# One tile of the fullest expert taken out of the plan and worked on while the last block is routed

## The reference

```python
h = x @ w_in                    # [2304, 2048]
x2 = (h - np.tanh(h)) @ w_out   # [2304, 512]
xn = x2 / (norm(x2) + 1e-6); en = expert_emb / (norm(expert_emb) + 1e-6)
logits = xn @ en.T / tau
expert_idx = np.argmax(logits, axis=1)
gate_w = softmax(logits)[arange(N), expert_idx]
for e in range(E):
    mask = expert_idx == e
    h = np.maximum(x2[mask] @ w1[e], 0.0)
    out[mask] = gate_w[mask, None] * (h @ w2[e])
```

## Time and profile before

| | us |
|---|---|
| median of 3 runs | 864.16 (864.05 to 864.76) |
| the profiled execution, its own time | 865.77 |
| its span | 863.6 |
| PE busy | 811.5 (94%) |
| DVE / ACT / POOL busy | 473.6 / 367.6 / 199.9 |

### The profile page before, as it was taken

How to read it: one execution, slowest core, us unless ns; L and a number is a source line. 1 busy time by engine, 2 the same in 40 slices (tenths; PEclk the granted TensorE clock), 3 DMA queues, 4 the chain that set the end, 5 groups by cost and what they waited for, 6 DMA issues and landing times. The chain is left out here.

```text
span 863.6 us, 16644 instructions
## 1 busy us (share of the span) xinstructions
PE 811.5 (94%) x4680; PEld 694.1 (80%) x4681; DVE 473.6 (55%) x1399; ACT 367.6 (43%) x910; POOL 199.9 (23%) x276
## 2 busy tenths in 40 slices
PE   7999999999999999999999999399999999999992
PEld 6888888888888888888888998377888888888871
DVE  7666655765577557755774565645533152545312
ACT  5554544433443344334432323325544262655433
POOL 4466521213121221221122000311112111111111
PEclk9999999999999999999999999589999999999996
DMA  9872123221322233222315110146461432566110
GB/s 173 232 233 62 38 50 98 74 60 48 97 68 64 49 87 82 62 49 70 85 26 219 61 50 1 38 120 246 140 218 53 146 134 80 193 231 221 48 43 20
DMA packets 106310, 87.87 MB, mean 102 GB/s; under 512 B 79012, under 2 KB 80169, under 8 KB 106242
## 3 DMA queue, kind: packets, MB, share of 16 engines
q1 hardware_dynamic: 98386, 74.92, 29.4%
q0 software_dynamic: 4624, 11.32, 4.2%
q10 hardware_dynamic: 3232, 0.79, 0.5%
HBM read 152.87 MB, written 11.46 MB: 190 GB/s over the span
## 5 line engine op out<-in xcount | busy, mean ns | idle before, releaser
L1259 PE MATMUL banks<-xh,win_h 128*128 128x384 f32 x384 | 135.5, 353 | 0.6 <-issue 0.6
L710 ACT CAST gh<-gf 128x384 fp32r<-128x384 f32 x96 | 49.2, 513 | 194.1 <-PE banks L1261 172.1
L958 DVE TENSOR_TENSOR gl<-gf,gh 128x384 fp32r<-128x384 f32 x96 | 59.2, 617 | 130.1 <-ACT gh L710 130.1
L1261 PE MATMUL banks<-xh,win_l 128*128 128x384 f32 x384 | 129.3, 337 | 0.0
L1260 PE MATMUL banks<-xl,win_h 128*128 128x384 f32 x384 | 129.1, 336 | 0.0
L1259 PE MATMUL banks<-wout_h,gh 128*128 128x512 f32 x288 | 119.8, 416 | 1.3 <-ACT x L719 1.3
L1260 PE MATMUL banks<-wout_l,gh 128*128 128x512 f32 x288 | 113.5, 394 | 0.0
L1261 PE MATMUL banks<-wout_h,gl 128*128 128x512 f32 x288 | 113.4, 394 | 0.0
L521 POOL TENSOR_TENSOR sm<-sm,rr 128x384 f32<-128x384 f32 x48 | 41.7, 869 | 273.3 <-DVE rr L883 273.2
L703 ACT ACTIVATE gf<-banks 128x384 f32<-128x384 f32 x96 | 46.9, 488 | 105.0 <-PE banks L1261 104.9
L1136 DVE TENSOR_TENSOR hTl<-banks,hTh 128x512 fp32r<-128x512 f32 x50 | 32.3, 686 | 92.1 <-ACT hTh L807 92.0
(11 more groups left out here) (192 smaller groups left out, 1513.5 us busy)
## 6 DMA issues: line engine op xcount, KB each, us to landing
w1raw<-in_moe_w_dram SPq DMA_DIRECT2D x104, 512.0 KB
w2raw<-in_moe_w_dram SPq DMA_DIRECT2D x104, 512.0 KB
x2T<-unit_embeddings SPq DMA_DIRECT2D x20, 256.0 KB, 3.6
junk<-unit_embeddings SPq DMA_DIRECT2D x20, 256.0 KB, 3.4
x_rows<-x SPq DMA_DIRECT2D x6, 768.0 KB, 5.1
wout_raw<-in_moe_w_out_dram SPq DMA_DIRECT2D x4, 1024.0 KB, 6.8
win_raw<-in_moe_w_in_dram SPq DMA_DIRECT2D x3, 1024.0 KB, 9.8
vw<-in_v_dram SPq DMA_DIRECT2D x16, 192.0 KB, 3.3
```

The source lines that it names most:

```text
L710: act.copy(gh[c % 2][:], gf[c % 2][:]).then_inc(g_high, 1)
L958: dve.tensor_tensor(gl[c % 2][:], gf[c % 2][:], gh[c % 2][:], ALU.subtract).then_inc(g_split, 1)
L1259: pe.matmul(to, sh, mh, start=start, stop=False)
L1261: return pe.matmul(to, sl, mh, start=False, stop=stop)
```

## The change

One tile, called the star in the code, leaves the plan. At c = 1 and 2 of the last block PE and DVE count the tokens of blocks 0 to 3 by expert and choose the fullest expert (`choose_star`; there are more than enough tokens for one full tile). SP then loads the first 128 rows of that expert's region of `table` and that expert's w1 and w2, where it loaded expert 0's before; POOL gathers the 128 rows of `x2` at c = 9, PE transposes them at c = 11, ACT and DVE split them at c = 12 and 13. ACT and DVE round and split the star's weights into slot 1, from c = 15 on and between the steps of the last routing; one piece of w2 is subtracted by POOL. PE makes the star's first product in pairs of pieces between the steps of the routing, and its hidden transposes and second product after the counts. Expert 0's w1 is loaded once the star's w1 is split, its w2 once the star's w2 is split. The plan gets one tile less (NTILE = 24), its start in the expert's region moved on by 128 rows (five more small DVE operations before `rows_planned`, one fewer after it). The star's output is scattered after the first two gathers.

```diff
-    NTILE = (T + E * (P - 1)) // P
+    NTILE = (T + E * (P - 1)) // P - 1
...
-        xh = sb("xh", [P, KC, 2, 2, GT], F32R, phase1)
+        xh = sb("xh", [P, 2, KC, 2, GT], F32R, phase1)
...
+        xg, xgh, xgl = [None, None], [None, None], [None, None]
+        for i in (1, 0):
...
-        psJ = banks[:, 0, :]
+        psJ = psXG_star = banks[:, 6, :]
+        psY_star = banks[:, 4, :]
...
-                if s == SLOTS * (NBLK - 1):
+                if s == SLOTS * (NBLK - 1) + 5:
                     sp.wait_ge(attended, NG)
-                    sp.wait_ge(table_cleared, 32)
-                    fetch_w1(None, 0, None)
-                    fetch_w2(None, 0, None)
+                    sp.wait_ge(star_chosen, 1)
+                    e = sp.value_load(star_int[0:1, 0:1], min_val=0, max_val=E - 1)
+                    sp.wait_ge(scattered, 16 * ST * (NBLK - 2))
+                    sp.dma_start(star_rows[:], table.rearrange("(n s) c -> n s c", s=P)[ds(e * MAXT, 1)].rearrange("n s c -> (n s) c")).then_inc(star_rows_loaded, 16)
+                    fetch_w1(None, e, None)
+                    fetch_w2(None, e, None)
                 if n > 0 and at == 7:
                     store(n - 1)
                 if n > 0 and at % 2 == 0 and 0 <= at // 2 - 1 < E:
                     load_en_row(n - 1, at // 2 - 1)
             store(NBLK - 1)
+            sp.wait_ge(star_w1_split, KC)
+            fetch_w1(None, 0, None)
+            sp.wait_ge(star_w2_split, KC - 1)
+            sp.wait_ge(star_w2_split_pool, 1)
+            fetch_w2(None, 0, None)
...
+                    if n == NBLK - 1 and c == 9:
+                        pool.wait_ge(star_ids_ready, 1)
+                        pool.wait_ge(h_ready, FC * (NBLK - 1))
+                        pool.wait_ge(x2_stored, 16 * (NBLK - 1))
...
             pool.wait_ge(squared, ST * NBLK)
             pool.tensor_tensor(norm[:], ss[:], power[:], ALU.pow).then_inc(rooted, 1)
+            pool.wait_ge(star_w2_high, 3)
+            pool.tensor_tensor(w2l4[:, ds(1, 1), 2, :].rearrange("p a f -> p (a f)"), w2raw[:, 2, :],
+                               w2h4[:, ds(1, 1), 2, :].rearrange("p a f -> p (a f)"), ALU.subtract).then_inc(star_w2_split_pool, 1)
             scatter_slots(NBLK - 1)
...
             gather(0, 0, 1)
+            pool.wait_ge(star_y_copied, 1)
+            pool.indirect_dma_start(out=out, out_offset=bass.IndirectOffsetOnAxis(ap=star_ids[:, 0:1], axis=0),
+                                    in_=star_y[:], in_offset=None, bounds_check=T - 1, oob_is_err=False).then_inc(star_y_stored, 16)
...
+            def star_round_w1(pieces):
+                round_w(w1raw, w1_loaded, w1h, ds(1, 1), star_w1_high, 16, pieces)
...
+                    if n == NBLK - 1 and c == FC - 1:
+                        star_round_w1([0])
                     high_g(n, c)
                     pieces(s + 1)
+                    if n == NBLK - 1 and c == 12:
+                        act.wait_ge(star_x_transposed, 1)
+                        act.copy(xgh[1][:], psXG_star.rearrange("p (k t) -> p k t", k=KC)).then_inc(star_x_high, 1)
...
-            round_w(w1raw, w1_loaded, w1h, ds(0, 1), w1_high, 16, [0, 1])
+            star_round_w1([1, 2, 3])
             wait(act, x2_stored, 16 * (NBLK - 1))
             act.wait_ge(dotted, ST * E * (NBLK - 1))
             for st in range(2):
                 act.wait_ge(acc_done, st + 1)
                 act.copy(x2[:, st, :], acc[st]).then_inc(acc_copied, 1)
             act.wait_ge(acc_copied, ST * NBLK)
+            act.wait_ge(star_x_split, 1)
             wait(act, rooted, NBLK - 1)
             for st in range(ST):
                 wait(act, squared, ST * (NBLK - 1) + st)
                 act.activation(psJ, x2[:, st, :], ACT.Square, accum_out=ss[:, st:st + 1]).then_inc(squared, 1)
+            def star_relu(half):
...
+            act.wait_ge(used, NBLK * FC)
+            round_w(w2raw, w2_loaded, w2h4, ds(1, 1), star_w2_high, 16)
+            star_relu(0)
             exp_gate(NBLK - 1)
-            round_w(w1raw, w1_loaded, w1h, ds(0, 1), w1_high, 16, [2, 3])
-            act.wait_ge(used, NBLK * FC)
-            round_w(w2raw, w2_loaded, w2h4, ds(0, 1), w2_high, 16)
+            star_relu(1)
+            for half in range(2):
+                act.wait_ge(star_hid_transposed, half + 1)
+                act.copy(hTh[:, half * KC:(half + 1) * KC, :], psHT[half].rearrange("p (k t) -> p k t", k=KC)).then_inc(star_hT_high, 1)
+            round_w(w1raw, w1_loaded, w1h, ds(0, 1), w1_high, 32)
+            act.wait_ge(star_y_ready, 1)
+            act.wait_ge(x2_stored, 16 * NBLK)
+            act.activation(star_y[:], psY_star, ACT.Copy, scale=star_rows[:, 1:2]).then_inc(star_y_copied, 1)
+            round_w(w2raw, w2_loaded, w2h4, ds(0, 1), w2_high, 32)
...
+            def choose_star():
...
+                then(dve.tensor_copy(count, psN))
...
+                then(dve.tensor_scalar(star[:], em8[:, 0, :], least, None, ALU.is_equal))
+                dve.tensor_scalar(star_int[:], least, float(E), None, ALU.add).then_inc(star_chosen, 1)
...
+            def star_low_w1(pieces):
...
+                    if n == NBLK - 1 and c == FC - 1:
+                        star_low_w1([0])
                     low_g(n, c)
                     pieces(s + 1)
+                    if n == NBLK - 1 and c == 2:
+                        choose_star()
+                    if n == NBLK - 1 and c == 6:
+                        dve.wait_ge(star_rows_loaded, 16)
...
+                    if n == NBLK - 1 and c == 13:
+                        dve.wait_ge(star_x_high, 1)
...
+            star_low_w1([1, 2])
             copy_acc(NBLK - 1)
+            star_low_w1([3])
             for st in range(ST):
                 dve.wait_ge(x2_transposed, st + 1)
                 if st == ST - 1:
                     dve.wait_ge(g_split, NBLK * FC)
                 dve.tensor_copy(x2T_last[st], psX_last[st]).then_inc(x2T_copied, 1)
+            star_low_w2([0, 1])
             choose(NBLK - 1, psL)
             place(NBLK - 1)
+            star_low_w2([3])
...
+            then(dve.tensor_tensor(left, tiles, star[:], ALU.subtract))
...
+            then(dve.tensor_scalar(started, starts, pcol[:, 0:1], None, ALU.is_le))
+            then(dve.scalar_tensor_tensor(out=started, in0=started, scalar=float(P), in1=star[:], op0=ALU.mult, op1=ALU.mult))
+            then(dve.tensor_tensor(jumped, jumped, started, ALU.add))
...
+            for half in range(2):
+                dve.wait_ge(star_hT_high, half + 1)
+                part = slice(half * KC, (half + 1) * KC)
+                dve.tensor_tensor(hTl[:, part, :], psHT[half].rearrange("p (k t) -> p k t", k=KC), hTh[:, part, :], ALU.subtract).then_inc(star_hT_split, 1)
...
+                    if n == NBLK - 1 and c == 1:
+                        pe.wait_ge(slotted, NBLK - 2)
+                        pe.matmul(psN, ones[:], running[:], start=True, stop=True).then_inc(star_counted, 1)
+                    if n == NBLK - 1 and c == 11:
+                        pe.wait_ge(star_gathered, 16)
...
+            def star_first(half, kk):
+                pe.wait_ge(star_x_split, 1)
+                pe.wait_ge(star_w1_split, kk + 1)
+                cols = slice(half * BANK, (half + 1) * BANK)
+                last = products(psG[half], (xgh[1][:, kk, :], xgl[1][:, kk, :]), [w[:, 1, kk, cols] for w in (w1h, w1l)], kk == 0, kk == KC - 1)
+                if kk == KC - 1:
+                    last.then_inc(star_hid, 1)
+            def star_transpose_hid(half):
...
+            def star_second():
+                pe.wait_ge(star_w2_split, KC - 1)
+                pe.wait_ge(star_w2_split_pool, 1)
...
+            star_first(0, 0)
+            star_first(0, 1)
             pe.wait_ge(acc_copied, ST * NBLK)
             for st in range(ST):
                 for kk in range(KC):
                     last = pe.transpose(psX_last[st][:, kk * P:(kk + 1) * P], x2[:, st, kk * P:(kk + 1) * P], ident[:])
                 last.then_inc(x2_transposed, 1)
+            star_first(0, 2)
+            star_first(0, 3)
             for st in range(ST):
                 pe.wait_ge(x2T_copied, st + 1)
                 for kk in range(KC):
                     last = pe.matmul(psL[:, st, :], x2T_last[st][:, kk * P:(kk + 1) * P], enT[:, kk, :], start=(kk == 0), stop=(kk == KC - 1))
                 last.then_inc(logits_ready, 1)
+            star_first(1, 0)
+            star_first(1, 1)
             rank(NBLK - 1)
+            star_first(1, 2)
+            star_first(1, 3)
             pe.wait_ge(slotted, NBLK)
             pe.matmul(psN, ones[:], running[:], start=True, stop=True).then_inc(totals_ready, 1)
+            star_transpose_hid(0)
+            star_transpose_hid(1)
+            star_second()
...
+            pe.wait_ge(star_y_copied, 1)
             transpose_xg(0, 0, 0)
             warm(4)
```

(8 more changed lines are left out.)

99 lines of the change are left out of this document (71 added, 28 removed).

## The result

The changed kernel takes 866.55 us (median of 15 executions, 864.51 to 869.24) against 864.64 (863.35 to 866.21) for the kernel before: a ratio of 1.0023 with a 95% interval of 1.0015 to 1.0032. It is slower; the forecast was 857.7, in a range of 854.1 to 861.0. In its profiled execution (866.18, span 864.4) the tile does go, and the hole grows by as much.

The account below looks back on a forecast made before the run. PE was taken as the bound: two full stretches and the routing hole between them. Removing a tile, -12.29, plus 5.8 for the later table (containing the block's 0.5) gave -6.5: 857.7 from 864.16, range 854.1 to 861.0.

Parts of the forecast that it names:

- The tile: Expert phase: one live tile of 22 goes, and all of its 12.29 us come back.
- The block: Last block, PE full: one matmul of the counts and four transposes added, +0.5 us.
- slower rival: Last block: star's weights delay the embedding row; landing to 497.2 costs nothing, at 503.7 the gain is gone; 866 or more, chance 0.05.
- Slots at 550.5: Last block's routing chain: with the star's work in it, slots are ready at 550.5 against 547.17, +3.35 us.
- nothing else of POOL's is late: Before the last block's scatters: POOL's w2 subtraction starts at 545.9 and is over by 549.4, delaying nothing else there.
- The scatters' landing: Last block's slot scatters beside expert 0's w2 load: 4.7 us at most when quiet, up to 6.2 beside loads; nothing to +1.5.
- the term for the scatter beside a subtraction: One slot scatter on POOL issued beside DVE's subtraction of 550.5 to 551.7: from nothing to +0.9 us.
- a table gather issued after 562 (scatters behind w2): Sign of being wrong, in the hole after the last block; the gather was forecast at 559.0 to 561.4.
- The second product at 564.0: Star's second product, ahead of the table transposes: starts 556.1 at half clock, full clock half way, ends 564.0; table taken 5.8 later.
- both are needed later: Expert 0's w1 rounded by 557 and w2 by 568.6, both before they are needed, so no cost.
- "hole grows more" rival: Hole: clock stays half or falls again, or scatters land later than 6.2 us behind w2; 859.2 to 862.4, chance 0.20.
- "no effect": The tile goes but the hole grows by 12 us, with the clock fallen twice; 862.4 to 865.9, chance 0.05.

Follow-up runs that it names:

- e6_pair: Changed kernel with expert 0's w2 load held until the table landed, POOL's w2 subtraction on DVE, two sets of `pair` and `slot` tiles; ratio 0.9960 to the kernel before.
- e1_hold_w2: Changed kernel with one wait added: expert 0's w2 is loaded only when all slot scatters have landed; ratio 0.9986 to the kernel before.
- e14_halves: e7_order with expert 0's w2 loaded in two halves, one in front of the slot scatters, one once the table has landed; ratio 0.9940 to the kernel before.
- e2_dve_w2: Changed kernel with POOL's one w2 subtraction given back to DVE, behind `place`; ratio 0.9982 to the kernel before.
- e7_order: e6_pair with the star moved forward: first-product pieces before the ranks, hidden transposes before the counts, their low part before the plan; ratio 0.9981 to the kernel before.
- e15_halves_pair: e6_pair with expert 0's w2 loaded in two halves, one in front of the slot scatters, one once the table has landed; ratio 0.9934 to the kernel before.
- e8_fill: e7_order with 18 matmuls that nobody reads in PE's two waits; ratio 0.9999 to the kernel before.
- e17_clock: e15_halves_pair with 17 matmuls of 512 columns that nobody reads, in front of the star's second product; ratio 0.9920 to the kernel before.

## Why the prediction was wrong

**The tile: right.** 12.29 forecast, 11.90 back, steps of 12.30 (631.61 to 643.91 between two row transposes). The 11.90 also hold two terms that nearly cancel: from tile 0's first product to tile 1's it is 8.08 instead of 8.88, as PE's granted clock was full there, and from tile 1's to tile 2's 14.33 instead of 13.45.

**The block: +0.5 was too little.** Its last second product starts at 538.76 instead of 538.10, +0.66; but this execution came to the last block early (block 3's slots at 468.98 instead of 469.54), so that the block took 1.22 longer. Of that PE waited 0.38 for the embedding row behind the star's weights, which landed at 497.27, at the edge of the 497.2 that was said to cost nothing; the other 0.84 is work added to the stream, where PE stood still nowhere else. In e6_pair's execution the row landed at 499.2 and cost 1.70, and in every kernel with the star it cost between 0.35 and 1.70. The mechanism of the slower rival is real; it did not decide.

**Slots at 550.5: 2.9 too early.** The one-hot came at 550.70 instead of 548.6, which is GpSimd's subtraction. The step that failed is "nothing else of POOL's is late": POOL was not late, but the prediction applied the shared port to GpSimd's scatter alone and not to the small operations of VectorE. The other part is the wait for `pair`, which the prediction did not name: block 4's scatters, themselves beside w1 and the store of `x2`, landed only at 552.1.

**The scatters' landing, "from nothing to +1.5": the step that turned the result.** It measured +6.32. The row it was taken from, 6.2 us at most, is of three scatters beside the load of the same weights in the middle of the dense part, and the largest of three was read as a bound. The gather went at 568.92, where the late bound was 561.4: of the 7.5 between them 4.8 are this term and 2.9 the slots, less 0.2 of the term for the scatter beside a subtraction. The prediction had put "a table gather issued after 562 (scatters behind w2)" among the signs of being wrong, and that sign came. The term for the scatter beside a subtraction was fine: 1.74 against 1.03 for the first one, and +0.72 for the three.

**The second product at 564.0.** It started at 559.00 (forecast 556.1, as `rows` were late), at half clock, got full clock back midway and took 8.46 (forecast 7.9). It ended at 567.5, and PE waited 3.87 more for the table. The clock stayed full until 551, as forecast, but the first-product pieces had ended at 547.8, and it fell behind the wait for the late ranks (3.03 us): the next pieces ran at half clock, 0.63 each. All of this lay under the table's lateness, so that the open point of the prediction, the clock, decided nothing here.

**Expert 0's w2, "both are needed later".** Right for expert 0, whose weights kept no product waiting. What the forecast did not see is that this load has small transfers on one side and the next expert's load, behind it on SP, on the other, which is issued at 588.91 instead of 575.70.

The "hole grows more" rival named 2 MB of w2 in the queues as a cause, and stopped at 862.4; "no effect" took two falls of the clock, not this. The right mechanism was listed twice, each time with too small a price.

## What to carry to other kernels

Where a chain of small transfers (scatter, gather, gather) is on the path, a weight load moved next to it cost 2 to 6 us a link here, and a hold only passes the cost to the next link; look for a place ahead of the chain, even for half of the load, and see what the issuing queue has behind it. Where a landing beside a load is on the path, the largest of a few that a trace shows is no upper bound (6.2 us there, 11.0 here). Work that GpSimd takes over in a stretch of small VectorE operations can hold one of them for all its length (2.3 us here).

## What the runs showed of the hardware

- Small indirect transfers beside 2 MB loads: the last block's three slot scatters landed in 6.3/8.9/11.0 us (min, median, max) in the changed kernel, against 3.2/3.4/4.7 with quiet queues; the table gather in 6.2 in e1_hold_w2, against 2.4 in the changed kernel. The Trainium skill (DMA: Bandwidth & Descriptors, Queues, rings and completion order) says that each DMA engine goes round between its queues packet by packet. How long a packet of the load holds an engine no run here shows, so whether that rule gives these microseconds stays open.
- A VectorE operation on 128x3 numbers took 2.31 to 2.35 us instead of 0.17 while a GpSimd subtraction of 128x1024 (2.33 to 2.67) ran, in every kernel that had one, and ended with it (548.59 and 548.57 in the changed kernel). No other small operation ran beside such a subtraction.
- PE's granted clock fell to 0.50 in the wait ahead of the star's second product or in that product's first matmuls, after waits of 2.69 (e14_halves) to 4.98 us (e2_dve_w2); over a wait of 2.69 e7_order kept it through the product (first matmul 0.47). It fell without any wait too: in e15_halves_pair at 546.7, right behind 2.7 us of logits of 8 columns, where the changed kernel kept it (first matmul 0.71 and 0.49). Where matmuls filled the waits it stayed full through the second product (e8_fill, e17_clock).
